# Attention and MLP kernel: banks and order of the first period changed, TensorE's attention loop written out

## The reference

```python
q_rot, k_rot = (rotate(q), rotate(k))            # rotary embedding
scores = scale * np.matmul(q_rot, k_rot.transpose(0, 1, 3, 2))
scores = scores - np.max(scores, axis=-1, keepdims=True)
attn = np.exp(scores)
attn = attn / (np.sum(attn, axis=-1, keepdims=True) + 1e-09)
attn_out = np.matmul(attn, v)                    # (4, 8, 576, 64)
x = attn_out.transpose(0, 2, 1, 3).reshape(2304, 512)
h = x @ w_in                                     # (512, 2048)
g = np.maximum(h, 0.0) + alpha * np.minimum(h, 0.0)
out = g @ w_out                                  # (2048, 512)
```

## Time and profile before

| | |
|---|---|
| median of 3 runs (lowest to highest) | 672.91 us (672.4 to 675.45) |
| the profiled execution | 672.58 us, its span 670.8 us |
| TensorE (PE) busy | 98% of the span |
| ScalarE, VectorE, GpSimd busy | 48%, 51%, 40% |
| mean granted TensorE clock | 0.997 |
| attention / MLP | to about 262 us / the rest |

### The profile page before, as it was taken

How to read it: one execution, slowest core, us unless ns; L and a number is a source line. 1 busy time by engine, 2 the same in 40 slices (tenths; PEclk the granted TensorE clock), 3 DMA queues, 4 the chain that set the end, 5 groups by cost and what they waited for, 6 DMA issues and landing times.

```text
span 670.8 us, 15166 instructions
## 1 busy us (share of the span) xinstructions
PE 656.0 (98%) x5570; PEld 561.7 (84%) x5570; DVE 338.8 (51%) x779; ACT 320.7 (48%) x730; POOL 266.8 (40%) x254
## 2 busy tenths in 40 slices
PE   8899999999999998999999999999999999999998
PEld 7677787777877776898899999999999999999996
DVE  4687777767888764445522332233233323332222
ACT  2788888868888875333332223222322232223223
POOL 3766788858865323222222222222222222222222
PEclk9999999989999999999999999999999999999999
DMA  6596554444554336000010001000100010001001
GB/s 148 153 229 178 124 136 110 106 105 103 120 121 104 83 117 251 1 1 1 1 48 0 1 1 47 1 1 0 47 0 0 0 47 0 0 0 48 1 0 48
DMA packets 73311, 41.62 MB, mean 62 GB/s; under 512 B 59812, under 2 KB 64292, under 8 KB 72740
## 3 DMA queue, kind: packets, MB, share of 16 engines
q1 hardware_dynamic: 72978, 40.62, 23.1%
q10 hardware_dynamic: 274, 0.16, 0.1%
HBM read 22.95 MB, written 4.72 MB: 41 GB/s over the span
## 4 chain that ended last, share of the span: by engine, by line
PE 94%; ACT 2%; DVE 1%; issue 1%; DMA 0%; SPq 0%; POOL 0%; ACTq 0%; DVEq 0%
PE banks L753 30%; PE banks L782 30%; PE banks L697 9%; PE banks L595 8%; PE banks L671 5%; PE banks L622 3%; PE banks L693 3%; PE banks L644 2%; PE banks L569 2%; PE banks L649 1%; ACT prob L824 1%; ACT pt L867 1%; DMA cos_sb<-in_cos 0%; PE banks L577 0%; PE banks L652 0%
## 5 line engine op out<-in xcount | busy, mean ns | idle before, releaser
L517 POOL TENSOR_TENSOR g_lo<-g,g_hi 128x384 fp32r<-128x384 f32 (+1 forms) x98 | 99.7, 1018 | 309.2 <-ACT g_hi L936 299.8
L1100 DVE TENSOR_SCALAR g<-banks,alpha_sb 128x384 f32<-128x384 f32 (+1 forms) x98 | 59.7, 610 | 250.9 <-ACT pos L927 250.9
L753 PE MATMUL banks<-x_hi,w_in_lo 128*128 128x384 f32 x384 | 129.3, 337 | 0.0
L753 PE MATMUL banks<-x_hi,w_in_hi 128*128 128x384 f32 x384 | 129.2, 337 | 0.0
L753 PE MATMUL banks<-x_lo,w_in_hi 128*128 128x384 f32 x384 | 129.0, 336 | 0.0
L927 ACT ACTIVATE pos<-banks 128x384 f32<-128x384 f32 x96 | 47.1, 491 | 170.2 <-PE banks L753 170.2
L782 PE MATMUL banks<-w_out_hi,g_hi 128*128 128x512 f32 x288 | 114.9, 399 | 0.3
L782 PE MATMUL banks<-w_out_hi,g_lo 128*128 128x512 f32 x288 | 112.9, 392 | 0.0
L782 PE MATMUL banks<-w_out_lo,g_hi 128*128 128x512 f32 x288 | 111.9, 388 | 0.0
L936 ACT ACTIVATE g_hi<-g 128x384 fp32r<-128x384 f32 (+1 forms) x98 | 50.9, 519 | 115.9 <-DVE g L1103 115.9
L824 ACT ACTIVATE prob<-prob,nmax 128x576 f32<-128x576 f32 x128 | 98.2, 773 | 1.3 <-DVE prob L991 1.2
(11 more groups left out here) (80 smaller groups left out, 917.3 us busy)
## 6 DMA issues: line engine op xcount, KB each, us to landing
q_swap<-q_nat SPq DMA_DIRECT2D x32, 256.0 KB, 3.7
k_swap<-k_nat SPq DMA_DIRECT2D x32, 144.0 KB, 3.1
out<-stage SPq DMA_DIRECT2D x18, 256.0 KB, 2.0
raw_q<-in_q SPq DMA_DIRECT2D x32, 128.0 KB, 2.9
raw_k<-in_k SPq DMA_DIRECT2D x32, 128.0 KB, 2.5
raw_v<-in_v SPq DMA_DIRECT2D x32, 128.0 KB, 2.3
w_in_raw<-in_moe_w_in SPq DMA_DIRECT2D x4, 1024.0 KB, 5.8
w_out_raw<-in_moe_w_out SPq DMA_DIRECT2D x8, 512.0 KB, 7.5
```

Of the source, the lines that this page charges most:

```text
L517: nc.gpsimd.tensor_tensor(g_lo[f % 2][:, part], g[f % 2][:, part], g_hi[f % 2][:, part].bitcast(F32), ALU.subtract).then_inc(g_lo_done, 1)
L753: mm = nc.tensor.matmul(h_ps[f % 2], w[:, j, cols], xx[:, j, :], start=(step == 0), stop=(step == 3 * CT - 1))
L1100: nc.vector.tensor_scalar(g[f % 2][:, part], h_ps[f % 2][:, part], 0.0, alpha_sb[:, f:f + 1], ALU.min, ALU.mult).then_inc(neg_done, 1)
```

## The change

The diff does four things. (1) In period 0 alone Q, K and MIXED take turn banks 2, 3 and 1 in place of 0, 1 and 2 (`bank_of`). (2) In period 0 alone MIXED moves behind score tile B3 on TensorE, behind the copy of PA1 on ScalarE, and behind maxima B4 on VectorE (`rank` keeps the counts right). `run_in` is left out ahead of B3 and B4, since its bank now holds K, and PA2 waits for K's evacuation. (3) TensorE's three batches after the first are written out: its attention has no hardware loop. The other engines keep theirs. (4) In the closing period VectorE does `split_x` ahead of the MIXED copy.

```diff
+OPENING_BANK = {U_Q: 2, U_K: 3, U_MIXED: 1}
...
+    def bank_of(p, u):
+        return OPENING_BANK.get(u, BANK_OF[u]) if isinstance(p, int) and p == 0 else BANK_OF[u]
+    def rank(p, u):
+        return U_PA[1] + 0.5 if p == 0 and u == U_MIXED else u
...
     def evac_count(p, u):
-        return tally(p, u, [w for w in range(UNITS) if BANK_OF[w] == BANK_OF[u]])
+        if isinstance(p, int):
+            return sum(exists(r, w) for r in range(-1, p + 1) for w in range(UNITS)
+                       if bank_of(r, w) == bank_of(p, u) and (r < p or rank(r, w) <= rank(p, u)))
+        return p * BANK_OF.count(BANK_OF[u]) + (evac_count(PAIRS, u) - PAIRS * BANK_OF.count(BANK_OF[u]))
...
-                if is_opening(p) and n > 1:
+                if is_opening(p) and A_TILES[0] < n <= B_TILES[1]:
                     run_in(1)
...
                 halves = (fill(p, u), fill(p, u + 1))
+                if u == U_PA[2] and is_opening(p):
+                    pe.wait_ge(evac[bank_of(p, U_K)], evac_count(p, U_K))
...
@@ TensorE, period
                     turn(p, t, U_Q)
                     turn(p, t, U_K)
-                    spread(p, t, U_MIXED)
                 spread(p, t, U_INV)
                 turn_two(p, t, U_PA[0])
                 score(p, t, B_TILES[2])
+                if is_opening(p):
+                    spread(p, t, U_MIXED)
                 score(p, t, B_TILES[3])
...
-            batches(pe, batch)
+            for b in range(NB):
+                batch(b)
@@ ScalarE, period
                 if is_opening(p):
-                    for u in OF_NEW:
-                        hi(p, u, t)
+                    hi(p, U_Q, t)
+                    hi(p, U_K, t)
...
                 flat(p, U_PA[1], t)
+                if is_opening(p):
+                    hi(p, U_MIXED, t)
                 flat(p, U_PA[3], t)
@@ VectorE, period
+                if not has_now(p):
+                    for j in range(CT):
+                        split_x(0, 0, j)
...
                 if not is_opening(p):
                     lo(p, U_MIXED, t)
-                if not has_now(p):
-                    for j in range(CT):
-                        split_x(0, 0, j)
...
                 if is_opening(p):
-                    for u in OF_NEW:
-                        lo(p, u, t)
+                    lo(p, U_Q, t)
+                    lo(p, U_K, t)
...
                 maxima(p, t, B_TILES[3])
+                if is_opening(p):
+                    lo(p, U_MIXED, t)
                 flat(p, U_PA[2], t)
```

More of the change, by code:

```diff
@@ L90, in exists_now @@
         return exists(PAIRS if not isinstance(p, int) else p, u)
+    def bank_of(p, u):
+        return OPENING_BANK.get(u, BANK_OF[u]) if isinstance(p, int) and p == 0 else BANK_OF[u]
+    def rank(p, u):
+        return U_PA[1] + 0.5 if p == 0 and u == U_MIXED else u
     def tally(p, u, counted):
         if isinstance(p, int):
-            return sum(exists(r, w) for r in range(-1, p + 1) for w in counted if r < p or w <= u)
+            return sum(exists(r, w) for r in range(-1, p + 1) for w in counted
+                       if r < p or rank(r, w) <= rank(p, u))
         return p * len(counted) + (tally(PAIRS, u, counted) - PAIRS * len(counted))
@@ L236, in by_rows @@
             else:
-                two = banks[:, 6:8, :] if u in (U_QREM, U_KREM) else banks[:, 4:6, :]
+                first = bank_of(p, U_QREM if u in (U_QREM, U_KREM) else min(U_Q, U_K, key=lambda w: bank_of(p, w)))
+                two = banks[:, 4 + first:6 + first, :]
                 first = (QT * D) * (u in (U_KREM, U_K))
@@ L357, in swap @@
                 if side == 0:
-                    sp.wait_ge(evac[BANK_OF[U_Q]], evac_count(p - 1, U_Q))
+                    sp.wait_ge(evac[bank_of(p - 1, U_Q)], evac_count(p - 1, U_Q))
                     dst, cols, arrived = q_swap[par], (slice(0, QT * P), slice(0, QT * P)), q_swap_in
@@ L361, in swap @@
                 else:
-                    sp.wait_ge(evac[BANK_OF[U_K]], evac_count(p - 1, U_K))
-                    sp.wait_ge(evac[BANK_OF[U_MIXED]], evac_count(p - 1, U_MIXED))
+                    sp.wait_ge(evac[bank_of(p - 1, U_K)], evac_count(p - 1, U_K))
+                    sp.wait_ge(evac[bank_of(p - 1, U_MIXED)], evac_count(p - 1, U_MIXED))
                     dst, cols, arrived = k_swap[par], (slice(0, HALF), slice(REM + HALF, REM + S)), k_swap_in
@@ L536, in fill @@
                 if not (isinstance(n, int) and n == 0):
-                    pe.wait_ge(evac[BANK_OF[u]], n)
-                return t_ps[BANK_OF[u]]
+                    pe.wait_ge(evac[bank_of(p, u)], n)
+                return t_ps[bank_of(p, u)]
             def turned_in(p, side):
@@ L560, in score @@
                     for u in OF_NEW:
-                        pe.wait_ge(evac[BANK_OF[u]], evac_count(p - 1, u))
+                        pe.wait_ge(evac[bank_of(p - 1, u)], evac_count(p - 1, u))
                 if not (isinstance(s, int) and s < 2):
@@ L685, in pv @@
                     for u in U_PB:
-                        pe.wait_ge(evac[BANK_OF[u]], evac_count(p, u))
+                        pe.wait_ge(evac[bank_of(p, u)], evac_count(p, u))
                 o = value_bank(p, h)
                 if o is o_last:
-                    pe.wait_ge(evac[BANK_OF[U_PB[1]]], evac_count(p, U_PB[1]))
+                    pe.wait_ge(evac[bank_of(p, U_PB[1])], evac_count(p, U_PB[1]))
                 elif not (isinstance(n, int) and n == 0):
@@ L768, in output @@
                         pe.wait_ge(exp_done, PERIODS * TILES)
-                        pe.wait_ge(evac[BANK_OF[U_PB[0]]], evac_count(PERIODS, U_PB[0]))
+                        pe.wait_ge(evac[bank_of(PERIODS, U_PB[0])], evac_count(PERIODS, U_PB[0]))
                     elif c == 2:
@@ L831, in hi @@
                 act.wait_ge(turned, unit_count(p, last_of(p, u)))
-                bank = t_ps[BANK_OF[u]]
+                bank = t_ps[bank_of(p, u)]
                 nx = (t + 1) % 2
@@ L867, in flat @@
                     ins = nc.scalar.activation(dst, src, ACT.Copy)
-                ins.then_inc(evac[BANK_OF[u]], 1)
+                ins.then_inc(evac[bank_of(p, u)], 1)
             def high_w_out(f):
@@ L1063, in normalise @@
                 if h == 0:
-                    dve.wait_ge(evac[BANK_OF[U_INV]], evac_count(p, U_INV))
+                    dve.wait_ge(evac[bank_of(p, U_INV)], evac_count(p, U_INV))
                 half = slice(h * HALF, (h + 1) * HALF)
```

## The result

The changed kernel took 669.14 us (median of 5 runs, 668.54 to 669.49), the kernel before 673.99 us (5 runs, 672.4 to 675.45). The ratio is 0.9923 (95% interval 0.9895 to 0.9952). The forecast was 670.4 us, the range 668.2 to 673.2. Run again in a later session, the changed kernel took 670.3 us (0.9940, 0.9918 to 0.9961). The profiled execution took 669.28 us with a span of 667.5 us.

The account below looks back on a forecast made before the run. TensorE (PE), busy for 98% of the span, was taken to bound the kernel. 672.58 - 3.95 (loop) + 1.6 (opening to period 2) + 0 (rest) = 670.2 us, median put at 670.4; range 668.2 to 673.2 us.

Parts of the forecast that it names:

- The loop: TensorE's attention loop, start of period 8: writing it out removes the 2.25 us gap and the clock loss behind it, -3.95 us.
- The 1.70 us for the clock: Period 8: half clock behind the branch's gap, taken as period 8's 16.50 us less period 9's 14.80, would go.
- the wait for PA1's copy: Period 0, TensorE: MIXED waits for ScalarE's copy of PA1, from 23.5 to 25.85, 2.35 us.
- k_swap's issue: Period 0, SyncE's queue: the two k_swap DMAs go out at 28.55 and 29.2, not from 25.33 on.
- GpSimd's late step: Period 0, GpSimd: its step waiting for MIXED starts at 26.3 in place of 22.77, 3.5 us later.
- Landed at 32.3, A1 at 32.4: Period 1: k_swap lands after a median 3.1 us and holds score tile A1, making TensorE 1.3 us late.
- rival B: Opening: the clock falls behind two gaps of 2.35 and 1.4 us, costing 1.7 us; 672.1 us, chance 10%.
- k_swap lands before PE wants it: Opening, ahead of A1 of period 1: stated sign that the prediction is wrong and the free-opening case holds.
- Pair 3's rope: GpSimd: rope of pair 3 ends at 49.3, not 46.55, so TensorE waits another 0.3 us (0 to 1.0).
- rival A: The opening costs nothing and the loop's whole 3.95 us stay gained: 668.4 to 668.7 us, chance 27%.
- C: MLP loop: the stall moves to its branch, costing 3.7 us; 674.1 us, slower than before, chance 7%.
- D: Attention: straight code must be fetched too and comes late, so writing out removes no wait; 674.2 us, chance 5%.

Follow-up runs that it names:

- one round in the loop: The kernel before, TensorE's attention loop going round once (batch 1 inside, batches 2 and 3 written out), no branch taken: 669.04 us, ratio 0.9932.
- the opening alone: The changed kernel with TensorE's attention loop kept and split_x in its old place, against the kernel before: 674.66 us, ratio 1.0017.
- The zeros: The changed kernel with 12 matmuls on zeros in the wait ahead of MIXED and 4 ahead of period 1: 671.89 us, ratio 0.9942.
- the slabs later: The changed kernel with PA1 copied first, plus w_in slab 0 sent in period 1, slabs 1 and 2 in period 2: 667.92 us, ratio 0.9894.
- the written-out kernel: The kernel before with TensorE's attention batches written out and nothing else: 669.16 us, ratio 0.9929; again 669.2 us, 0.9926.

## Why the prediction was right, and where it was not

**The loop.** The place and the cause were right: no gap at period 8, no branch, and no blocks fetched anew. The term was mis-sized: 3.95 us were forecast and 5.21 us measured. By period of the kernel before, over the 14.73 us that a period takes when written out: 2.67 us in period 7 (the gap and 0.4 us around it), 1.58 us in period 8 (the clock), and 0.96 us spread over periods 4, 5, 6, 9, 10 and 11. I had taken period 9, itself in the loop, as the measure of an undisturbed one. The 1.70 us for the clock came from windows that aren't cut at the starts of periods: by PE's timeline period 8 took 16.31 us and period 9 14.81, 1.50 us less. With one round in the loop only 0.2 us of such spread was left; what the rest is, I did not settle. The clock's fall, which I had as a firm term, is not bound to this gap: the opening alone had a branch of 4642 ns, a gap of 2.54 us and no fall behind it, and its loop still cost 4.66 us.

**Period 0.** MIXED ahead of B4, the wait for PA1's copy, the 0.75 us of low parts, k_swap's issue and GpSimd's late step all came in the order forecast and within 0.5 us, of which 0.35 us is the earlier start. "Landed at 32.3, A1 at 32.4" failed in its first half: the DMAs took 2.5 us, not the median of 3.1, and landed at 31.2. A1 still came at 32.0, but for another reason: rival B had come true, two gaps of 2.81 and 1.14 us and 6.8 us of half clock behind them. By the prediction's own words it is wrong where k_swap lands before PE wants it, and it did. The step that failed is the clock, put at nothing in the sum and given 10% because the 2.18 us of gap in the profile of before had cost none; in three other executions the same gap was followed by 3.4 or 6.8 us at half clock. Period 3 came 2.48 us later after the first score, not 1.6. The zeros show that these costs do not add: with the clock held, k_swap and the rope hold TensorE in its place, 0.75 us at A1.

**Pair 3's rope.** Forecast 49.3 and 0.3 us of waiting, measured 49.63 and 0.24 us. In the four other executions of this opening there was no such wait.

**The sum.** -5.21 and +2.48 with -0.55 us of start-up and end give -3.3 us; the forecast had -3.95 and +1.6, -2.35. The two errors have opposite signs, so the total came nearer than its parts, and that is luck. The medians differ by 4.85 us, more than the profiled executions. The clocks suggest why: the kernel before was profiled at a mean clock of 0.997, with one fall, while 35 of its 41 runs beside the experiments have 0.995 or less. The forecast was 0.37% less, the ratio says 0.77% less; the median of before had moved from 672.91 to 673.99 us, which also brought the absolute time nearer. From 672.91 us the ratio would have given 667.7 us, under the range.

**The chances.** The measured 669.14 us is 0.72% under the median of before, which is "faster"; that had 32% against 64% for "within 0.5%". The time came near rival A's (668.4 to 668.7 us) by another way than A's: the opening was not free, the loop was dearer. C and D did not happen: the MLP's branch kept its 238 ns, and the straight periods have no such wait. On that the Trainium skill (Runtime: NRT & Kernel Launch, Instruction fetch mechanics) agrees with the trace in kind: it expects a fetch and a wait where a taken branch leads to code no longer held. Two blocks were fetched at the attention's branch and none at the MLP's, and of the two taken branches the one of 4 periods cost 4.4 to 4.6 us, the one of two chunks 0.24 us. No run here varied a loop's length, so where the limit lies was not tried; by the blocks, a loop of five was held and one of about seven (59 us at a block every 8 us, an estimate) was not.

**A better version.** Two have lower medians, by different ways, both with the attention written out: the old opening with zeros in its gap (667.83 us), and the new opening with PA1 copied first (668.09 us; with the slabs later 667.92 us). The second is shown to be faster. With PA1 copied first it beat the written-out kernel on one chip. With the slabs later it shared a chip with the changed kernel, and its five runs (666.47 to 668.5 us) lie below all seven of that one (669.5 to 672.49 us).

## What to carry to other kernels

Where one engine is busy 98% of the time, look at its sequencer's rows at loop ends, and at the instruction queue beside them: one taken branch, with two blocks fetched anew, was the whole gain here, and the other loop's, with none, cost nothing. When a unit is moved later, follow its last reader into every queue that waits for it; here MIXED held TensorE, SyncE's k_swap and GpSimd's rope at once. Take the price of an undisturbed stretch from a stretch that is really undisturbed, and the price of the clock from more than one execution.

## What was not expected of the hardware

TensorE stood at 1.2 GHz for 6.8 us in four and 10.2 us in one profiled execution behind one and the same pair of gaps (2.8 us, then 0.8 to 1.1), for 0 or 6.8 us behind gaps of 1.3 and 1.1 us, and for 0, 3.4 or 6.8 us behind a gap of 2.2 us. So one kernel's time spreads: on one chip the mean clock of the kernel before was 0.997 in its run of 672.59 us and 0.985 in that of 678.3 us. With zeros in the one long gap of the opening it was 1.000 in four runs of six. The same k_swap DMA took 2.5 us to land with nothing ahead of it in the queue, and 3.7 to 3.8 us right behind q_swap.
